# Clamping three chunks of alpha on ScalarE, with steps of the first sequence on VectorE, ScalarE and the load queue put in another order

## The reference

```
state = alpha[:, :, t, :, None] * state + k[:, :, t] (outer) v[:, :, t]     # per head, 768 steps
y[:, :, t] = q[:, :, t] @ state
x  = y as rows of (4, 768, 384)
x  = x + relu(layer_norm(x) * g_ln @ w_ch1) @ w_ch2                            # first MLP, 384 -> 1536 -> 384
u  = x + real(fft(fft(x, axis=1), axis=2))
out = u + relu(layer_norm(u) @ w_ch1') @ w_ch2'                                # second MLP
```

## Time and profile before

| | |
|---|---|
| median of 3 executions | 792.6 us (792.46 to 798.22) |
| profiled execution | 792.46 us |
| its span | 791.0 us, 1.46 us less than its time |
| TensorE busy | 782.1 us, 99% |
| VectorE busy | 468.0 us, 59% |
| ScalarE busy | 214.5 us, 27% |
| GpSimd busy | 55.3 us, 7% |

### The profile page before, as it was taken

One profiled execution on the slowest core, in us unless ns is written; L12 is line 12 of the kernel. 1 busy time (PEld: TensorE's weight loads), 2 busy tenths in 40 slices (PEclk: granted clock), 3 DMA queues, 4 the chain that ended last, 5 costly groups with the idle time before them and its releaser, 6 DMA issues.

```text
span 791.0 us, 13706 instructions
## 1 busy us (share of the span) xinstructions
PE 782.1 (99%) x5426; PEld 765.2 (97%) x5426; DVE 468.0 (59%) x1049; ACT 214.5 (27%) x424; POOL 55.3 (7%) x109
## 2 busy tenths in 40 slices
PE   8999999999999999999999999999999999999998
PEld 7998999999999999999999999999999999999998
DVE  7988585856667476577486775437543564342422
ACT  3543232232312322223234333112221232111211
POOL 1000000000000000000001300210012000300000
PEclk9999999999999999999999999999999999999999
DMA  9343113031130420431323511120002100000000
GB/s 253 120 139 88 49 56 112 31 106 62 37 99 31 107 70 31 126 106 45 130 71 100 180 70 51 41 101 31 1 31 86 45 0 18 12 1 31 0 31 31
DMA packets 29814, 53.89 MB, mean 68 GB/s; under 512 B 1916, under 2 KB 24700, under 8 KB 29756
## 3 DMA queue, kind: packets, MB, share of 16 engines
q1 hardware_dynamic: 29756, 53.10, 21.4%
HBM read 43.65 MB, written 13.37 MB: 72 GB/s over the span
## 4 chain that ended last, share of the span: by engine, by line
PE 86%; issue 6%; DVE 5%; ACT 1%; POOL 1%; DMA 0%; POOLq 0%; DVEq 0%
PE h L95 12%; PE acc L97 12%; PE acc L95 12%; PE acc L96 12%; PE h L97 11%; PE h L96 11%; PE side_bank L1393 4%; PE side_bank L1349 2%; PE side_bank L1383 2%; PE side_bank L1401 2%; PE side_bank L96 2%; PE side_bank L97 2%; PE side_bank L95 1%; PE side_bank L1363 1%; PE side_bank L1333 1%
## 5 line engine op out<-in xcount | busy, mean ns | idle before, releaser
L169 DVE SCALAR_TENSOR_TENSOR hT_low<-h,hT_high 128x384 fp32r<-128x384 f32 (+1 forms) x204 | 108.5, 532 | 178.7 <-ACT hT_high L164 178.0
L95 PE MATMUL h<-xnT_high,w_high 128*128 128x384 f32 (+1 forms) x612 | 205.4, 336 | 1.4 <-DVE hT_low L169 1.4
L97 PE MATMUL h<-xnT_high,w_low 128*128 128x384 f32 (+1 forms) x612 | 199.4, 326 | 0.0
L96 PE MATMUL h<-xnT_low,w_high 128*128 128x384 f32 (+1 forms) x612 | 199.3, 326 | 0.0
L95 PE MATMUL acc<-w_high,hT_high 128*128 128x384 f32 x576 | 194.0, 337 | 0.0
L164 ACT ACTIVATE hT_high<-h 128x384 fp32r<-128x384 f32 (+1 forms) x204 | 96.3, 472 | 359.4 <-PE h L97 359.2
L97 PE MATMUL acc<-w_high,hT_low 128*128 128x384 f32 x576 | 192.9, 335 | 0.0
L96 PE MATMUL acc<-w_low,hT_high 128*128 128x384 f32 x576 | 192.5, 334 | 0.0
L95 PEld LDWEIGHTS h<-xnT_high,w_high 128*128 128x128 f32 x612 | 115.2, 188 | 5.0 <-DVE hT_low L169 1.7
L96 PEld LDWEIGHTS h<-xnT_low,w_high 128*128 128x128 f32 x612 | 115.3, 188 | 0.0
L97 PEld LDWEIGHTS h<-xnT_high,w_low 128*128 128x128 f32 x612 | 115.0, 188 | 0.0
(11 more groups left out here) (123 smaller groups left out, 768.6 us busy)
## 6 DMA issues: line engine op xcount, KB each, us to landing
stage<-w_dram SPq DMA_DIRECT2D x24, 384.0 KB, 3.6
x_scratch<-x_unit SPq DMA_DIRECT2D x8, 576.0 KB, 3.3
a_in<-alpha_dram SPq DMA_DIRECT2D x6, 672.0 KB, 5.1
q_in<-q_dram SPq DMA_DIRECT2D x6, 672.0 KB, 7.5
k_in<-k_dram SPq DMA_DIRECT2D x6, 672.0 KB, 8.7
v_in<-v_dram SPq DMA_DIRECT2D x6, 576.0 KB, 3.8
xb<-x_scratch SPq DMA_DIRECT2D x4, 576.0 KB, 4.2
xb<-x_turned SPq DMA_DIRECT2D x4, 576.0 KB, 6.8
```

The lines of the kernel that those rows point to most:

```text
L95: pe.matmul(out, wh, xh, start=start, stop=False)
L96: pe.matmul(out, wh, xl, start=False, stop=False)
L97: return pe.matmul(out, wl, xh, start=False, stop=stop)
L169: dve.scalar_tensor_tensor(out=self.hT[1][:, j % H_SLOTS, 0:u.cols], in0=self.hps[j % H_BANKS][:, 0:u.cols], scalar=0.0, in1=self.hT[0][:, ...
```

## The change

- Chunks 3, 4 and 5 of alpha are clamped by ScalarE: three relus one behind the other, `relu(1.25 - x)`, `relu(0.5 - that)`, `relu(that + 0.75)`, at steps 4, 8 and 10 of unit `ONE[0]`. VectorE did chunk 3 at step 3 of `ONE[0]`, and chunks 4 and 5 at slots 0 and 2 in unit `ONE[1]`. Each clamped chunk has a semaphore of its own.
- SP loads chunk 4 behind weight piece 4, ahead of pieces 5 to 11. It did so behind piece 11.
- `next_state` of chunk 2 (first of `ONE[1]`) goes from VectorE's step 6 to step 8.
- `prepare_k(ONE[3], 0)` and `prepare_k(ONE[4], 0)` go from slot 11 to the slot of `prepare_q`, 6 and 7.
- `ONE[2].range_slot` is no longer set to 1 and has the class's 4.
- Two `keep_clock(2)` of the start-up become `keep_clock(5)` and `keep_clock(6)`; GpSimd writes two more constants.

```diff
-ONE[2].next_slot, ONE[2].rows_slot, ONE[2].range_slot = 6, 7, 1
+ONE[2].next_slot, ONE[2].rows_slot = 6, 7
...
-ONE[2].next_k_slot = ONE[3].next_k_slot = JH - 1
...
             def load_again(g):
                 s = g - UT
-                sp.wait_ge(a_bounded, s + 1)
+                sp.wait_ge(clamped[s], 1)
...
-                sp.wait_ge(a_bounded, u.base)
+                if u.n == 3:
+                    for g in range(UT, CHUNKS):
+                        sp.wait_ge(clamped[g], 1)
+                else:
+                    sp.wait_ge(a_bounded, u.base)
...
-            split.dma(sp, ONE_W[PIECES:])
+            split.dma(sp, ONE_W[PIECES:5])
             load_again(4)
+            split.dma(sp, ONE_W[5:])
...
-            for i, limit in enumerate((-A_HIGH, A_LOW)):
+            for i, limit in enumerate((-A_HIGH, A_LOW, A_HIGH, A_HIGH - A_LOW)):
...
+            def clamp(g):
+
+                done = 2 * (g - UT)
+                act.wait_ge(first_a[g], 16)
+                act.wait_ge(F_inv_ready, g - UT + 1)
+                to = a_safe[:, g % UT, :]
+                act.activation(to, a_in[:, g % UT, :], ACT.Relu, bias=limits[:, 2:3], scale=-1.0).then_inc(clamp_step, 1)
+                act.wait_ge(clamp_step, done + 1)
+                act.activation(to, to, ACT.Relu, bias=limits[:, 3:4], scale=-1.0).then_inc(clamp_step, 1)
+                act.wait_ge(clamp_step, done + 2)
+                act.activation(to, to, ACT.Relu, bias=limits[:, 1:2]).then_inc(clamped[g], 1)
...
                 side_one(ONE[1], j)
+                if j in (4, 8, 10):
+                    clamp({4: 3, 8: 4, 10: 5}[j])
...
-                if u.n == 2 and slot in (0, 2):
-                    bound_chunk(UT + 1 + slot // 2)
...
                     prepare_q(following, 0)
-                if slot == u.next_k_slot and slot < JH - 1 and following:
                     prepare_k(following, 0)
...
-                if slot == u.next_k_slot == JH - 1:
-                    prepare_k(following, 0)
...
                 if j == 3:
                     prepare_k(u, 0)
-                    bound_chunk(3)
...
                     prepare_q(u, 1)
                     prepare_k(u, 1)
+                if j == 8:
                     next_state(u, 0)
-                if j == 8:
                     split.low(dve, ONE_W[9])
...
-            keep_clock(2)
+            keep_clock(5)
             outputs(ONE[0], 0)
-            keep_clock(2)
+            keep_clock(6)
```

More of the change, by code:

```diff
@@ L51, in __init__ @@
         self.q_slots, self.k_slots = {0: 1, 3: 2}, {2: 1, 4: 2}
-        self.next_slot, self.next_k_slot, self.rows_slot, self.range_slot = 7, 7, 9, 4
+        self.next_slot, self.rows_slot, self.range_slot = 7, 9, 4
     def first(self):
@@ L308, in pipeline @@
             head_rows = sb1("head_rows", [R, 2])
-            limits = sb1("limits", [R, 2])
+            limits = sb1("limits", [R, 4])
             act_warm = sb1("act_warm", [R, 1])
@@ L363, in pipeline @@
         a_bounded = sem("a_bounded")
+        clamped = [sem(f"clamped{g}") for g in range(CHUNKS)]
+        clamp_step = sem("clamp_step")
         above_checked = sem("above_checked")
@@ L612, in _ @@
             pool.memset(state[:, :, :, :, :], 0.0).then_inc(s_ready, 1)
-            pool.wait_ge(consts_done, 4)
+            pool.wait_ge(consts_done, 6)
             def inv_std(u, rows=None):
@@ L736, in _ @@
         def _(act):
+            def clamp(g):
[8 more added lines that the diff above has]
+                act.activation(to, to, ACT.Relu, bias=limits[:, 1:2]).then_inc(clamped[g], 1)
+                if g == CHUNKS - 1:
+                    act.wait_ge(clamped[g], 1)
+                    act.sem_inc(a_bounded, CHUNKS)
             def check_range(u):
@@ L826, in side_dim @@
                     sin_up(n, slot // 2)
-            act.wait_ge(consts_done, 4)
+            act.wait_ge(consts_done, 6)
             act.activation(act_warm[:, :], limits[:, 0:1], ACT.Copy)
@@ L928, in bound_chunk @@
                 dve.wait_ge(first_a[g], 16)
[L929 to L932, removed]
+                dve.tensor_scalar(a_safe[:, g, :], a_in[:, g, :], A_LOW, A_HIGH,
+                                  ALU.max, ALU.min).then_inc(clamped[g], 1)
             def bound_alpha(u):
@@ L941, in scan_forward @@
                 s, g = u.slot(c), u.base + c
-                dve.wait_ge(a_bounded, g + 1)
+                if u.b == 0:
+                    dve.wait_ge(clamped[g], 1)
+                else:
+                    dve.wait_ge(a_bounded, g + 1)
                 if g >= UT:
```

## The result

| | before | after |
|---|---|---|
| median | 792.58 us (10 executions) | 803.84 us (10 executions, 802.15 to 806.23) |
| span of the profiled execution | 791.0 us | 802.7 us |
| TensorE busy | 782.1 us | 788.8 us |

The ratio after to before is 1.012, 95% interval 1.009 to 1.015: slower by 11 us. The forecast was 797.7 us, range 793.5 to 801.5. Three of the ten executions before took about 798.2 us, the other seven 792.3 to 792.7.

What follows compares the result with a forecast made beforehand. TensorE, busy 782.1 of 791.0 us, was taken as the bound: 0.2 + 0 + 2.0 - 0.5 + 2.5 - 0.5 + 1.5 = +5.2 us gave 796.2, with 1.46 around it 797.7; range 793.5 to 801.5.

Steps and rivals of the forecast that it cites:

- the clock falls: Rival: TensorE falls to half pace behind new gaps, up to 2.5 us each; 800.2 for one, 805 for three; chance 0.15.
- The three waits: Terms for new TensorE waits at transpose_k of chunk 3, pe_up(9) of ONE[1], and the transposes of ONE[3]'s rows.
- +2.0: next_state of chunk 2 behind step 8's low part: TensorE waits 2.0 us at transpose_k; +1.3 to +2.3.
- +2.5: Range check at slot 4: late alpha delays pe_up(9) of ONE[1]; low end 1.0, 3.5 if k lands 2 us later.
- +1.5: prepare_k for ONE[4] moved ahead of a low part: statistics and transposes at 136.97 come 1.5 us later; +1.0 to +2.0.
- The two gains: -0.5 for two clamps less on VectorE in ONE[1]; -0.5 for prepare_k of ONE[3] out of slot 11, TensorE's wait at 105.21.
- Start-up: TensorE's 3 and 4 added identity matmuls delay outputs and scores(1); term +0.2, between 0 and +0.4.
- Weights and the load of chunk 4: Loads ahead of pieces 5 and 6: piece 6 split 0.4 us later, about when TensorE asks; term 0, up to +1.
- The ends of the sum: Total with the low or high ends of all terms, given as 794.5 to 800 us.

Runs made afterwards that it cites:

- the filled waits: Changed kernel with 8, 12 and 9 identity matmuls that TensorE runs ahead of its three long waits; 799.26 us, median of 6.
- the kernel with three back: Changed kernel with range check of ONE[2] at slot 1, next_state of chunk 2 at step 6, prepare_k(ONE[4], 0) at slot 11; 792.81 us.
- the run with the check back: Changed kernel with the range check of ONE[2] back at slot 1; 797.51 us, median of 10.
- the best kernel: Changed kernel with range check, next_state, prepare_k(ONE[4], 0) and load order as before, added identity matmuls kept; 791.74 us, ratio to before 0.998.

## Why the prediction was wrong

- **The step that failed** is the one that put the clock's fall at a chance of 0.15 and left it out of the sum. The forecast took TensorE's waits to cost one for one, since gaps of 0.63 us in the one trace had brought nothing. Waits of 1.90, 2.87 and 2.16 us cost a low stretch of 1.7 us each besides, 5.1 us together, and the filled waits show that the idleness alone did it. That trace was of a common execution; the one of 798.22 us in the table before was a sign that something can bring such a loss in this kernel too. The prediction thinks of it beside the start-up's gaps, but not where it sets the chance of a fall.
- **The rival** *the clock falls* had the right mechanism and gave 805 for three falls; 803.84 was measured. Its price per fall, 2.5 us from the first stretch of the kernel, was too high: a low stretch was mostly 3.4 us and cost 1.7. It named the wait at `pe_up(9)` as the one that decides; in the profiled execution all three did. The Trainium skill, *TensorE: Matmul & The Clock Gate*, section "Part 1: The HAM clock gate", says that half rate is the default state and that activity releases it. The trace agrees, with a granted clock of 0.50 at each of the three waits. I had that rule and the waits side by side and trusted the small gaps of the trace instead.
- **The three waits** were right in place and cause: +2.0 against 1.90 measured; +2.5 against 2.87; +1.5 against 2.16 - 0.61 = 1.55. In the second the size is partly luck. Alpha landed after 4.8 us, not 5.3, and by the rows of the changed kernel the wait would have been 2.87 - 1.07 = 1.8 us; k landed after 10.1 us, not 8.4, and was not there 0.9 us early, as the sum had it, but 1.07 late, as the high end allowed. The Trainium skill, *DMA: Bandwidth & Descriptors*, section "Anatomy of one DMA", gives the formula that the prediction quotes for transfers issued by GpSimd; these are SP's, so its 3.6 us was no forecast for them.
- **The two gains** of 0.5 came: the waits of 0.52 and 0.49 are gone, the small one of 0.20 stays.
- **Start-up**, +0.2: 0.2 in the kernel before with only these matmuls added.
- **Weights and the load of chunk 4**, term 0, up to +1: mis-sized. It is +0.4 alone and 1.1 in the kernel with three back; TensorE waited 0.24 to 1.25 us at `pe_up(6)` in the profiles that have this load order. On ScalarE piece 6 began at 36.19 to 37.26 us in these eight profiles, 1.8 to 2.9 later than the 34.35 of the earlier trace rows, where the prediction had about one. The clamp took 2.2 us for three passes, where it had 1.9.
- **The ends of the sum** are added up wrongly: the high ends of all terms give 792.46 + 8.8 = 801.3, not 800. It changes nothing, since the clock is in none of them.

With the clock and 0.4 for the weights, the sum is 797.7 + 5.1 + 0.4 = 803.2.

## What to carry to other kernels

On a kernel whose TensorE is hardly ever idle, add up not only the length of each new wait but the stretch at half clock that may follow it, and where the wait can't be avoided, fill it with matmuls that nobody reads. Ask of a late load what stands between it and the next thing that the bound engine wants: here the 2.5 us of `prepare_k` and its wait for k made the difference between no wait and one of 2.87 us. Look at the spread of a kernel's times before trusting its median; a second cluster 5.7 us up was, in the kernel where one of its executions was profiled, a clock that fell in the start-up.

## What the hardware showed that I had not expected

- A wait of 1.90 us was enough to bring TensorE from 2.4 to 1.2 GHz for 3.4 us (once 6.8), and not always: the wait of 2.17 us at 141 us in the run with the check back brought nothing. A longer wait brought no longer stretch: 3.4 us behind 3.28 us as well.
- In the start-up, with short matmuls of 48 and 128 columns around them, waits of 0.63 us and less went with a fall in 5 of 12 executions, and the clock stayed down for some 14 us; in the body of the kernel a wait of 1.25 us in the profile of one run did nothing. Nor did one of 0.70 us at 9.5 us, in the start-up of the best kernel.
- The granted clock prints 1.00 from the span's start, also where the first 24 identity records took 5.0 us and the next 24 took 2.5.
- Three loads of 672 KB, issued by SP within 0.8 us, landed far apart in the changed kernel: alpha 4.8 us after its issue, k 10.1 us after its own.
